# Row weights of an attention stage by DMA through DRAM in place of on-chip transposes, and GpSimd's weight splits moved within the pair

## The reference, cut to what matters

```python
def _attn_ref(q, k, v, M_prev, z_prev, beta):          # B, H, S, D = 4, 8, 576, 64
    scores = (1 / sqrt(D)) * q @ k^T, causal mask
    a = exp(scores - rowmax);  a /= a.sum(-1) + 1e-9
    local = a @ v
    q_p = phi(q)                                        # elu(q) + 1
    mem_out = (q_p @ M_prev) / ((q_p . z_prev) + 1e-6)
    g = sigmoid(beta)                                   # per head
    return g * mem_out + (1 - g) * local

x = attn_out.transpose(0, 2, 1, 3).reshape(2304, 512)   # tokens x features
h = x @ w_in1;  g = 0 if h <= -1, h if h >= 1, else (h + 1)**2 / 4;  x = g @ w_out1    # 512 -> 2048 -> 512
h = x @ w_in2;  g = h * sigmoid(h);                                  out = g @ w_out2
```

## Time and profile before

| what | value |
|---|---|
| median of 3 runs | 986.52 us (985.75 to 989.36) |
| profiled execution, its own time | 986.77 us |
| its span in the profile | 984.6 us |
| PE busy over the span | 974.2 us |
| DVE, ACT, POOL busy | 478.4, 384.0, 286.0 us |
| mean granted TensorE clock | 0.999 |
| attention stage | the first 192 us of the span |
| DMA queue q1 | 38336 packets, 47.20 MB |

### The profile page before, as it was taken

One profiled execution on the slowest core, in us unless ns is written; L12 is line 12 of the kernel. 1 busy time (PEld: TensorE's weight loads), 2 busy tenths in 40 slices (PEclk: granted clock), 3 DMA queues, 4 the chain that ended last, 5 costly groups with the idle time before them and its releaser, 6 DMA issues.

```text
span 984.6 us, 14130 instructions
## 1 busy us (share of the span) xinstructions
PE 974.2 (99%) x5468; PEld 814.4 (83%) x5468; DVE 478.4 (49%) x946; ACT 384.0 (39%) x847; POOL 286.0 (29%) x304
## 2 busy tenths in 40 slices
PE   8999999999999999999999999999999999999998
PEld 6888778888888888888888998888888888888897
DVE  7999999756344434434344663323332332322232
ACT  7988888633223222322223332322222232222222
POOL 7999999799000000000000798000000000000000
PEclk9999999999999999999999999999999999999999
DMA  6555454244000000000000343001000100100010
GB/s 213 152 161 157 145 145 141 60 128 117 12 1 1 1 0 1 1 1 1 1 1 1 87 133 92 0 1 43 1 1 1 44 0 1 43 1 1 1 44 22
DMA packets 38401, 48.10 MB, mean 49 GB/s; under 512 B 3264, under 2 KB 21696, under 8 KB 38336
## 3 DMA queue, kind: packets, MB, share of 16 engines
q1 hardware_dynamic: 38336, 47.20, 16.0%
HBM read 42.47 MB, written 4.72 MB: 48 GB/s over the span
## 4 chain that ended last, share of the span: by engine, by line
PE 89%; DVE 6%; ACT 2%; issue 1%; DMA 0%; POOL 0%; SPq 0%; POOLq 0%
PE ps L1020 26%; PE ps L1022 26%; PE ps L1021 26%; PE ps L953 3%; PE ps L898 3%; PE ps L861 2%; DVE prob L652 1%; PE ps L973 1%; PE ps L877 1%; DVE glo L796 1%; ACT prob L475 1%; DVE qlo L634 1%; DVE rw L684 1%; PE ps L939 1%; PE ps L946 1%
## 5 line engine op out<-in xcount | busy, mean ns | idle before, releaser
L1020 PE MATMUL ps<-xhi,W 128*128 128x512 f32 (+1 forms) x640 | 235.5, 368 | 0.0
L1021 PE MATMUL ps<-xlo,W 128*128 128x512 f32 (+1 forms) x640 | 235.4, 368 | 0.0
L1022 PE MATMUL ps<-xhi,W 128*128 128x512 f32 (+1 forms) x640 | 235.4, 368 | 0.0
L796 DVE TENSOR_TENSOR glo<-act_t,ghi 128x512 fp32r<-128x512 f32 (+1 forms) x160 | 118.1, 738 | 223.5 <-ACT ghi L575 223.5
L575 ACT CAST ghi<-act_t 128x512 fp32r<-128x512 f32 (+1 forms) x160 | 92.5, 578 | 235.4 <-PE ps L1022 213.1
L1020 PEld LDWEIGHTS ps<-xhi,W 128*128 128x128 f32 x640 | 120.6, 188 | 20.7
L1021 PEld LDWEIGHTS ps<-xlo,W 128*128 128x128 f32 x640 | 120.6, 188 | 20.6
L1022 PEld LDWEIGHTS ps<-xhi,W 128*128 128x128 f32 x640 | 120.6, 188 | 20.0
L335 POOL CAST W<-stage 128x512 fp32r<-128x512 f32 x64 | 49.1, 767 | 303.0 <-PE ps L1022 300.6
L567 ACT ACTIVATE act_t<-act_t,half_col 128x512 f32<-128x512 f32 (+1 forms) x80 | 54.5, 681 | 185.7 <-DVE act_t L789 185.7
L1020 PE MATMUL ps<-ghi,W 128*128 128x512 f32 (+1 forms) x320 | 118.1, 369 | 0.2
(11 more groups left out here) (113 smaller groups left out, 1334.9 us busy)
## 6 DMA issues: line engine op xcount, KB each, us to landing
stage<-in_moe_w_in SPq DMA_DIRECT2D x32, 256.0 KB, 2.7
stage<-in_moe_w_out SPq DMA_DIRECT2D x32, 256.0 KB, 2.7
vn<-in_vN SPq DMA_DIRECT2D x16, 320.0 KB, 4.5
qraw<-in_qT SPq DMA_DIRECT2D x15, 320.0 KB, 3.4
qn<-in_qN SPq DMA_DIRECT2D x16, 288.0 KB, 4.1
zb<-in_zN SPq DMA_DIRECT2D x32, 144.0 KB, 3.8
out_x<-ostage SPq DMA_DIRECT2D x17, 256.0 KB, 2.0
kraw<-in_kT SPq DMA_DIRECT2D x15, 288.0 KB, 3.0
```

What stands on the lines that cost most here:

```text
L796: nc.vector.tensor_tensor(glo[:, f % SLOTS, 0:TN[tile]], a, ghi[:, f % SLOTS, 0:TN[tile]].bitcast(F32), ALU.subtract).then_inc(glo_done, 1)
L1020: nc.tensor.matmul(dst, w_lo_, x_hi_, start=first, stop=False)
L1021: nc.tensor.matmul(dst, w_hi_, x_lo_, start=False, stop=False)
L1022: return nc.tensor.matmul(dst, w_hi_, x_hi_, start=False, stop=last)
```

## The change

POOL's `widen`, PE's `turn_row` and its matmul on line 933, and ACT's `empty_row` and half of `empty_rest` are gone, and rwide with them. In their place SP writes rw[:, 0] of the pair to a DRAM buffer `rows_at` (one DMA, `send_rows`), laid so that a score block's 128 rows follow each other, and reads it back (four DMAs, `spread_rows`) into turned[:, 1], each row of weights copied to the 64 partitions of its head. DVE's second reciprocal waits for the send of the pair before, to_x for the four landings. The matmuls of T_PHI go to bank 2 of PSUM and no longer to the ring of two. In POOL's turn the pieces of weights are split behind weigh and ahead of phi_sum_2.

```diff
-        RING = [T_M1, T_M20, T_M31, T_TAIL, T_PHI, T_ROW]
-        AMONG_SCORES = {T_M0: 2, T_M30: 0, T_M21: 1, T_REST: 3}
+        RING = [T_M1, T_M20, T_M31, T_TAIL]
+        AMONG_SCORES = {T_M0: 2, T_M30: 0, T_M21: 1, T_REST: 3, T_PHI: 2}
...
+            def send_rows(p):
+                sp.wait_ge(row_step, 4 * p + 2)
+                if p >= 2:
+                    sp.wait_ge(row_in, 64 * (p - 1))
+                sp.dma_start(rows_at[p % 2].rearrange("c r -> r c"), rw[:, 0, :],
+                             allow_slow_non_contiguous=True).then_inc(row_out, 16)
+
+            def spread_rows(p):
+                sp.wait_ge(row_out, 16 * (p + 1))
+                sp.wait_ge(x_free, p + 1)
+                for e in range(2):
+                    part = slice(e * D, (e + 1) * D)
+                    by_block = rows_at[p % 2, 0:2 * FULL].rearrange("(m e) r -> e m r", e=2)[e:e + 1]
+                    sp.dma_start(turned[part, 1, 0:MAIN].rearrange("p (m r) -> p m r", m=FULL),
+                                 by_block.broadcast_to([D, FULL, P])).then_inc(row_in, 16)
+                    sp.dma_start(turned[part, 1, MAIN:S],
+                                 rows_at[p % 2, 2 * FULL:, part].broadcast_to([D, D])).then_inc(row_in, 16)
...
                     load_m(p + 1)
+                send_rows(p)
+                spread_rows(p)
                 for u in parts_beside(p):
                     fetch(u + 2)
...
                 weigh(p)
-                widen(p)
+
+                for u in parts_beside(p):
+                    split_part(u)
 
                 if 0 < p < NPAIR - 1:
                     phi_sum_2(p + 1)
...
-                for u in parts_beside(p):
-                    split_part(u)
...
-                nc.scalar.copy(turned[:, :, MAIN:S],
-                               ring(p, T_REST)[:, 0:P].rearrange("p (w n) -> p w n", w=2)).then_inc(ev_act, 1)
+                nc.scalar.copy(turned[:, 0, MAIN:S], ring(p, T_REST)[:, 0:D]).then_inc(ev_act, 1)
...
-            def empty_row(p):
...
                 if step == 1:
                     if p:
-                        dve.wait_ge(t_full, TURNS * p)
+                        dve.wait_ge(row_out, 16 * p)
...
                 dve.wait_ge(values_done, p + 1)
-                dve.wait_ge(ev_act, len(BY_ACT) * (p + 1))
+                dve.wait_ge(row_in, 64 * (p + 1))
...
-                elif u == T_REST:
+                elif u in (T_REST, T_PHI):
                     if p + 1 < NPAIR:
                         pe.wait_ge(s_read, NB * (p + 1) + 6)
+                    else:
+                        pe.wait_ge(ev_act, len(BY_ACT) * p + BY_ACT.index(T_M0) + 1)
...
-                last = nc.tensor.matmul(to[:, D:P], rwide[:, 2 * FULL:, :], sident[:], start=True, stop=True)
...
-            def turn_row(p):
```

More of the change, by code:

```diff
@@ L100, in build @@
         rw = sb("rw", [P, 2, NB], where=att)
-        rwide = sb("rwide", [P, 2 * FULL + 2, D], where=att)
         rwt = sb("rwt", [P, 2, 2], where=att)
@@ L118, in build @@
         ostage = sb("ostage", [P, 2, BANK])
+        rows_at = nc.dram_tensor("rows_at", (2, NB, P), F32).ap()
         ps = ctx.enter_context(nc.psum_tensor("ps", [P, 8, BANK], F32))
@@ L145, in score_at @@
             return BANK * (U_BANK[U_OF[s]] + e) + (P if s == 1 else 0), keys(s)
-        TURNS = 10
-        T_M0, T_M1, T_M20, T_M30, T_M21, T_M31, T_TAIL, T_REST, T_PHI, T_ROW = range(TURNS)
-        RING = [T_M1, T_M20, T_M31, T_TAIL, T_PHI, T_ROW]
-        AMONG_SCORES = {T_M0: 2, T_M30: 0, T_M21: 1, T_REST: 3}
-        BY_ACT = [T_M0, T_M20, T_M30, T_M31, T_TAIL, T_REST, T_PHI, T_ROW]
+        TURNS = 9
+        T_M0, T_M1, T_M20, T_M30, T_M21, T_M31, T_TAIL, T_REST, T_PHI = range(TURNS)
+        RING = [T_M1, T_M20, T_M31, T_TAIL]
+        AMONG_SCORES = {T_M0: 2, T_M30: 0, T_M21: 1, T_REST: 3, T_PHI: 2}
+        BY_ACT = [T_M0, T_M20, T_M30, T_M31, T_TAIL, T_REST, T_PHI]
         BY_DVE = [T_M1, T_M21]
-        LAST_BANK = {T_PHI: 0, T_ROW: 1}
-        LAST_PRIOR = {T_PHI: T_M30, T_ROW: T_M21}
         def ring(p, u):
-            if p == NPAIR - 1 and u in LAST_BANK:
-                return ps[:, LAST_BANK[u], :]
             if u in RING:
@@ L169, in emptied @@
             q, v = g // len(RING), RING[g % len(RING)]
-            if p == NPAIR - 1 and u in LAST_PRIOR:
-                q, v = p, LAST_PRIOR[u]
             if v in BY_ACT:
@@ L188, in build @@
         phi_part, phi_sum, phi_norm = sem("phi_part"), sem("phi_sum"), sem("phi_norm")
-        norm_step, row_step, row_wide = sem("norm_step"), sem("row_step"), sem("row_wide")
+        norm_step, row_step = sem("norm_step"), sem("row_step")
+        row_out, row_in = sem("row_out"), sem("row_in")
         weighed, v_done = sem("weighed"), sem("v_done")
@@ L372, in weigh_v @@
                                         ALU.mult).then_inc(v_done, 1)
[L374 to L380, removed]
             def weigh(p):
@@ L497, in empty_rest @@
                 act.wait_ge(t_full, TURNS * p + T_REST + 1)
-                act.wait_ge(x_free, p + 1)
-                nc.scalar.copy(turned[:, :, MAIN:S],
-                               ring(p, T_REST)[:, 0:P].rearrange("p (w n) -> p w n", w=2)).then_inc(ev_act, 1)
+                nc.scalar.copy(turned[:, 0, MAIN:S], ring(p, T_REST)[:, 0:D]).then_inc(ev_act, 1)
             def empty_phi(p):
@@ L504, in empty_phi @@
                 nc.scalar.copy(turned[:, 0, 0:MAIN], ring(p, T_PHI)).then_inc(ev_act, 1)
-            def empty_row(p):
-                act.wait_ge(t_full, TURNS * p + T_ROW + 1)
-                nc.scalar.copy(turned[:, 1, 0:MAIN], ring(p, T_ROW)).then_inc(ev_act, 1)
             phi_part_1(0)
@@ L546, in _ @@
                 empty_phi(p)
-                empty_row(p)
                 if not more:
@@ L929, in turn_rest @@
                 pe.wait_ge(weighed, 2 * p + 2)
-                pe.wait_ge(row_wide, 2 * p + 1)
                 to = ring(p, T_REST)
-                nc.tensor.matmul(to[:, 0:D], phs[:, 2 * FULL:, :], sident[:], start=True, stop=True)
-                last = nc.tensor.matmul(to[:, D:P], rwide[:, 2 * FULL:, :], sident[:], start=True, stop=True)
-                last.then_inc(t_full, 1)
+                nc.tensor.matmul(to[:, 0:D], phs[:, 2 * FULL:, :], sident[:], start=True, stop=True).then_inc(t_full, 1)
             def turn_phi(p):
@@ L1012, in _ @@
                 turn_phi(p)
-                turn_row(p)
                 first_values(p)
```

## The result

The changed kernel takes 1104.9 us (1101.08 to 1107.77, 4 runs) against 987.75 us: 1.119 times the time before, 95% interval 1.117 to 1.121. The forecast was 994.5 us with a range up to 1018. The direction was right, the size was off by a factor of 15: 8 us more were forecast, 117 measured.

The account below looks back on a forecast made before the run. PE was taken to bound turns without a weight piece, POOL and DVE those with one. Eleven turns +6.3 us, other turns +2, last pairs giving back 0.5: +8 on 984.6, forecast 994.5 us, range 977 to 1018.

Parts of the forecast that it names:

- What bounds the kernel: Attention pair loop: PE sets turns without a weight piece (11.00 us), POOL and DVE those with one (12.10 us).
- fully hidden work: Attention stage, all new work hidden: eleven turns gain 7.2 us, the five other pairs 2 in all, together 9 us.
- What is moved: Weight pieces split earlier in POOL's turn: at most 1.5 us over five turns, half of that in the sum.
- The tie on high_k: POOL's high_k and DVE's low_k both come near 5.4 us behind rwt; at most 0.3 us late in five turns.
- L1: Landing of send_rows on SP, from its issue: 3.2 us of queue plus 2.9 of packets, 6.1 us, between 4.4 and 10.0.
- 3.2 us of queue ahead: DMA queue: packets of v, q and z ahead of the send clear 2.4 to 4.3 us after its issue, 3.2 taken.
- upper bound of 10.0: Dearest landing of the send: 4.3 us of queue plus 5.7 us of packets at 78 ns each.
- The loop on SP: SP's round of loads, send, wait and spreads takes 5.7 us plus L1: turns of 11.8 us, 12.25 with a piece.
- to_x as the weaker limit: DVE's to_x needs 10.7 us from the send's issue; late only if the turn is shorter than about 11.1 us.
- The tail: Last pair's send and spreads land by 193.7 to 194.7 us: no cost, about 1 us with 78 ns per packet.
- Rival 3: Send's 4-byte writes much dearer, landing 10.0 us, turns 15.7 and 16.2, total 1047 us; chance 0.12 of over 1016.
- Rival 1: Send back within 4.8 us and hidden; PE sets 10.5 us, POOL 11.15; 977.5 us; chance 0.27 of over 0.5% faster.

Follow-up runs that it names:

- experiment 8: Changed kernel without send, spreads and their waits, row weights left out and the output multiplied with 1.0: 981.6 us, ratio 0.995 to the kernel before.
- experiment 1: Kernel before with only the weight pieces moved, split behind weigh and widen in POOL's turn: 987.2 against 987.3 us, ratio 1.000.
- experiment 6: Changed kernel with five sends differing in number and spacing of 4-byte writes, spreads reading z behind the same wait: 987.5 to 1067.5 us.
- experiment 5: Changed kernel with the send kept but no wait on SP, spreads reading z, reciprocals alternating between two buffers: 1032.2 us, ratio 1.045.

## Why the prediction was right or wrong

**What bounds the kernel:** right for PE and POOL with DVE as a pair; but I took DVE's 10.00 us of busy time as room down to 10.5, and in a turn with a piece took POOL's 0.9 us off 12.06 although DVE was busy for 11.67 of it. DVE's operations can stretch when POOL is beside them (1.01 for 0.17 us), and experiment 8 shows turns of 10.94 us with everything removed. A turn with a piece and one without, from to_x to the second to_x behind it, took 22.9 us together and take 21.9 there: 1.0 us less and not 0.55 + 0.9. The gain for fully hidden work, priced at 9 us, measures 5.5.

**What is moved:** priced at 0.75 us, measured 0 (experiment 1). The tie on high_k did become a wait, of DVE for khi in five turns (2.0 us in all, at most 0.5), which the total does not show.

**The step that failed** is "Landing L1 = 3.2 + 2.9 = 6.1 us after the issue, between 4.4 and 10.0". It measures 11.4 us in the profiled run (9.8 to 13.5 over its sixteen sends). The 3.2 us of queue ahead were fair: the small packets begin to run some 2.5 us behind the send's issue. Their number was exact too: q1 has 29952 packets more than before, 1872 a pair, which is the 1168 of the send and 704 for the four spreads. The term for their time was wrong in kind. I priced the time for which packets occupy the engines, from three rows that all showed just that the earlier trace rows; it turned out less than the lowest of them, 14 ns and not 40. What I had no term for is the time between the last packet and the semaphore, 8 us here and 7.6 in the median. None of the rows could show it, because every DMA in the kernel before moves runs of 48 bytes and more, and its only writes to DRAM are of 2048. The upper bound of 10.0 came from dearer packets, which did not occur, and did not hold either. The Trainium skill's line in "DMA: Bandwidth & Descriptors", section "Specifications", that below 512 bytes the engine reads, modifies and writes, pointed at the right place; I gave it no chance of its own beside the sum. The crowding of experiment 6 agrees with such a mechanism without showing it.

**The loop on SP** was right in structure and nearly in size: 5.7 + L1 was forecast, with 0.2 for fetches; 7.0 to 7.4 + L1 is measured in nine runs. The missing 1.3 us are issues: the spreads 0.65 and not 0.57 apart, n 0.62, k 0.48 and q 0.47 and not 0.37 each, and now and then one of 1.1 to 2.3 us. By the loop and the measured landing the turn would have been 17.3 us; the profile has 18.7. With the earlier trace rows's 11.39 as the turn of before, thirteen turns of 18.7 lose 95 of the 105.5 us.

**to_x as the weaker limit:** right; it waits in every turn, but only because the turn is the landing's.

**The tail:** forecast at nothing to 1 us, measured 9.2: the landing again (11.4 for the send instead of 4.5 to 5.5), and 3 us of it because PE came back from its idle time at the lower clock, for which I had no term.

**Rival 3**, dearer writes, is the case that happened, with a chance of 0.12 for anything over 1016 us and a price of 1047; its mechanism was per packet, and its price half of the loss. That it named the right case is in part luck. Rival 1 was not to be had at 977.5 us in any version.

## What to carry to other kernels

A DMA that is waited for costs its completion, not its packets: look at the gap between the last packet and the wait's end, and never price a write whose element size has no row in the trace by rows of larger ones. Transposing by a strided DMA write of 4-byte elements onto neighbouring addresses was the most expensive of the ways tried to turn 4.6 KB around; one small transpose on PE and runs of 512 bytes did the same with no loss (986.9 and 982.9 us against 986.3 and 986.9 before). And before a wait is put at the head of a queue that also carries all loads, add up the whole round of that queue: issues, landing, issues again.

## What the runs showed of the hardware that I had not expected

1152 writes of 4 bytes on neighbouring addresses left the DMA engines in about a microsecond (14 ns each) and were confirmed 8 us later; at a distance of 64 bytes the same number was confirmed 1.1 us behind the last packet. Transfers queued behind unconfirmed small writes landed in 8 to 11 us instead of 3 to 5 (experiment 5), and their packets took 525 ns instead of 111. The same program showed medians of 10.8 and 11.4 us for this landing in two sets of runs, 13 us of total time apart, while the kernel before repeated within 0.2%. And SP's issue of an ordinary DMA, 0.3 to 0.6 us, stretched to between 1.1 and 2.3 us six times before 300 us in the changed kernel; what it waits for then was not found.
